# Splitting the weighted sum of a half head into two groups of six matmuls instead of three groups, in a clustered attention kernel

## The reference

```python
mask = q_assign[:, :, :, None] == k_assign[:, :, None, :]
scores = scale * np.matmul(q, k.transpose(0, 1, 3, 2))
scores = np.where(mask, scores, -1000000000.0)
scores = scores - np.max(scores, axis=-1, keepdims=True)
attn = np.exp(scores)
attn = attn / (np.sum(attn, axis=-1, keepdims=True) + 1e-09)
x = np.matmul(attn, v)          # then (token, head*dim)
h = x @ w_in;  x = (h * (1.0 / (1.0 + np.exp(-1.702 * h)))) @ w_out          # 512 -> 2048 -> 512
h = x @ w_in2; solu = h * softmax(h); out = (layernorm(solu) * g) @ w_out2   # 512 -> 1024 -> 512
```

## Time and profile before

| | |
|---|---|
| median of 3 runs | 654.56 us |
| lowest, highest | 654.29, 655.52 us |
| the profiled execution | 655.62 us, of which the span 653.8 us |
| mean granted clock of TensorE in it | 0.997 of full speed |
| busy: PE, PEld, DVE, ACT, POOL | 97%, 81%, 71%, 55%, 69% of the span |

### The profile page before, as it was taken

One profiled execution on the slowest core, in us unless ns is written; L12 is line 12 of the kernel. 1 busy time (PEld: TensorE's weight loads), 2 busy tenths in 40 slices (PEclk: granted clock), 3 DMA queues, 4 the chain that ended last, 5 costly groups with the idle time before them and its releaser, 6 DMA issues.

```text
span 653.8 us, 11249 instructions
## 1 busy us (share of the span) xinstructions
PE 632.8 (97%) x3269; PEld 531.8 (81%) x3269; DVE 465.5 (71%) x796; ACT 357.6 (55%) x712; POOL 451.1 (69%) x587
## 2 busy tenths in 40 slices
PE   7899999999999999999999999999999999999998
PEld 4488989899898988888878888788888888788876
DVE  3789999999999975646445766854556578778660
ACT  2689999999999875333334343353332154443341
POOL 3697879798798796766667777766666776857000
PEclk9989999999999999999999999999999999999999
DMA  8945454554544601233323322333330000000001
GB/s 307 288 131 140 115 146 110 144 131 107 149 118 109 227 2 65 97 97 96 96 96 96 96 90 83 94 90 93 96 96 32 1 0 18 33 18 17 33 32 49
DMA packets 26122, 62.75 MB, mean 96 GB/s; under 512 B 3697, under 2 KB 9841, under 8 KB 26097
## 3 DMA queue, kind: packets, MB, share of 16 engines
q1 hardware_dynamic: 24368, 59.30, 31.3%
q10 hardware_dynamic: 1728, 3.15, 1.3%
HBM read 46.51 MB, written 4.72 MB: 78 GB/s over the span
## 4 chain that ended last, share of the span: by engine, by line
PE 68%; ACT 11%; issue 7%; DVE 5%; POOL 4%; DMA 2%; SPq 1%; DVEq 1%; ACTq 0%; POOLq 0%
PE banks L587 7%; PE banks L602 7%; PE banks L604 7%; PE banks L603 7%; PE banks L617 7%; PE banks L619 7%; PE banks L618 6%; ACT probs L856 4%; PE banks L572 4%; ACT probs_th L867 3%; DMA pair_t<-k_t 2%; PE banks L744 2%; PE banks L742 2%; PE banks L743 2%; ACT x_sums L873 2%
## 5 line engine op out<-in xcount | busy, mean ns | idle before, releaser
L1090 DVE TENSOR_TENSOR probs_tl<-banks,probs_th 128x384 fp32r<-128x384 f32 x192 | 100.6, 547 | 10.6 <-ACT probs_th L867 7.2
L1070 DVE TENSOR_REDUCE neg_max<-banks 128x1 f32<-128x768 f32 x96 | 91.2, 950 | 6.4 <-PE banks L559 4.5
L867 ACT CAST probs_th<-banks 128x384 fp32r<-128x384 f32 x192 | 83.1, 486 | 18.8 <-PE banks L572 17.4
L1383 POOL TENSOR_TENSOR wait_scrap<-half_power 128x1 f32<-128x1 f32 x126 | 26.0, 206 | 97.3 <-PE banks L619 66.8
L856 ACT ACTIVATE probs<-banks,neg_max 128x768 f32<-128x768 f32 x96 | 88.2, 919 | 2.4 <-DVE neg_max L1070 2.3
L1459 POOL TENSOR_SCALAR probs<-probs,row_inv 128x768 f32<-128x768 f32 x96 | 87.6, 913 | 0.0
L1064 DVE TENSOR_TENSOR gl<-gate,gh 128x512 fp32r<-128x512 f32 x48 | 40.3, 840 | 63.4 <-ACT gh L841 63.4
L572 PE MATMUL banks<-ident,probs 128*128 128x128 f32 x576 | 80.0, 275 | 0.1
L587 PE MATMUL banks<-probs_th,v_parts 128*128 128x384 f32 x192 | 70.4, 366 | 9.0 <-DVE x_sums L1097 9.0
L1442 POOL TENSOR_TENSOR downl<-gelu_raw,downh 128x512 fp32r<-128x512 f32 x48 | 76.0, 1582 | 4.0
L617 PE MATMUL banks<-gh,downh 128*128 128x512 f32 x192 | 76.0, 396 | 0.4 <-POOL downl L1442 0.2
(11 more groups left out here) (166 smaller groups left out, 1431.5 us busy)
## 6 DMA issues: line engine op xcount, KB each, us to landing
gelu_raw<-w_gelu SPq DMA_DIRECT2D x48, 512.0 KB, 3.5
ln_raw<-w_ln SPq DMA_DIRECT2D x8, 512.0 KB, 4.0
pair_t<-q_t SPq DMA_DIRECT2D x4, 768.0 KB, 9.2
pair_t<-k_t SPq DMA_DIRECT2D x4, 768.0 KB, 11.6
v_raw<-v_r SPq DMA_DIRECT2D x16, 192.0 KB, 2.4
out<-gelu_raw ACTq DMA_DIRECT2D x12, 256.0 KB, 2.0
kq_raw<-k_t SPq DMA_DIRECT2D x14, 192.0 KB, 3.3
kq_raw<-q_t SPq DMA_DIRECT2D x14, 192.0 KB, 3.4
```

The lines of the kernel that those rows point to most:

```text
L867: nc.scalar.copy(probs_th[half % 2][:, c * CH:(c + 1) * CH, i * P:(i + 1) * P], pt_bank(n, c).rearrange("p (t s) -> p t s", t=CH)).then_in ...
L1070: nc.vector.tensor_reduce(out=neg_max[:, col], in_=scores[n % 2], op=ALU.max, axis=mybir.AxisListType.XY, negate=True).then_inc(max_done, 1)
L1090: nc.vector.tensor_tensor(probs_tl[half % 2][at], pt_bank(n, c).rearrange("p (t s) -> p t s", t=CH), probs_th[half % 2][at].bitcast(F32), ...
```

## The change

Two edits, both of order alone; no instruction is added or taken away.

1. The twelve matmuls come in two groups of six. The first group stands behind S_b (before: three behind S_a, five behind S_b), the second behind T_c and ahead of S_c (before: four there).
2. The first head's two transfers of cluster rows are issued ahead of the second head's two.

```diff
-            for x in range(2):
-                for j in range(2):
+            for j in range(2):
+                for x in range(2):
                     first_cluster_rows(j, x)
...
-            HEAD_SPLIT = (0, 3, 8, 12)
+            HEAD_SPLIT = (0, 6, 12)
+            HEAD_STEPS = (HEAD_LAG + AHEAD + 1, HEAD_LAG + AHEAD + 2)
+
             def head_half(it, n, c):
...
-                    for c, lag in enumerate(HEAD_LAG + AHEAD + c for c in range(3)):
-                        if c in (2,) and exists(it, n, lag, STEPS) and (n - lag) % CH == CH - 1 and not (
-                                drain and n >= lag):
-                            head_half(*lagged(it, n, lag, STEPS), c)
+                    lag = HEAD_STEPS[1]
+                    if exists(it, n, lag, STEPS) and (n - lag) % CH == CH - 1 and not (drain and n >= lag):
+                        head_half(*lagged(it, n, lag, STEPS), 1)
                     if not drain:
                         scores_of(it, n)
-                    for c, lag in enumerate(HEAD_LAG + AHEAD + c for c in range(3)):
-                        if c in (0, 1) and exists(it, n, lag, STEPS) and (n - lag) % CH == CH - 1 and not (
-                                drain and n >= lag):
-                            head_half(*lagged(it, n, lag, STEPS), c)
+                    lag = HEAD_STEPS[0]
+                    if exists(it, n, lag, STEPS) and (n - lag) % CH == CH - 1 and not (drain and n >= lag):
+                        head_half(*lagged(it, n, lag, STEPS), 0)
```

## The result

| | before | after |
|---|---|---|
| median | 654.80 us (654.29 to 655.52, 4 runs) | 659.27 us (659.09 to 659.60, 4 runs) |
| the profiled execution's span | 653.8 us | 657.0 us |
| first `x_sums` to last in the loop (28 periods) | 188.25 us | 191.38 us |
| from there to the last `x_sums` of the attention | 20.20 us | 20.67 us |

The changed kernel takes 1.0068 times as long as before (95% interval 1.0051 to 1.0085), 4.5 us more. That is slower by more than a measurement's uncertainty, and inside the range that the prediction gave to its own case (658.5 to 663 us); the 5.6 us forecast were 1.1 us too many.

A forecast was written before the change was run, and what follows sets the result against it. The prediction took a closed loop of waits in the attention, from `x_sums` to `x_sums`, as the bound. Loop 4.6 plus ends 0.4 and 0.5, with 0.05 and roundings, gave 5.6 us: 660.2 us against the median, range 656.0 to 664.0.

The forecast's parts named there:

- its own case: Whole kernel: the loop of waits lengthens and the ends add, 5.6 us slower; range 658.5 to 663 us, chance 0.70.
- The term of the loop: Attention loop: 28 periods x 0.165 us longer, 4.6 us; lower bound 3.1 us if the short offset holds in each half head.
- What bounds: Attention: one closed loop of waits from `x_sums` to the next `x_sums`, 6.70 us, sets the whole period.
- The wait that takes the place of the removed one: T_b's second group on TensorE: waits for `probs_tl` in place of `x_sums`, some 28 times, 0.5 us each.
- `x_sums` to S_b: Loop piece without the three matmuls: 1.40 to 1.51 us instead of 1.81, mean gain 0.355 us.
- S_b to S_c: Loop piece with twelve matmuls instead of nine: 3.52 us instead of 3.00, three matmuls costing 0.52 us.
- The ends: Outside the loop: first half head plus 0.4 us, last steps plus 0.52 us.
- First half head: Ahead of the loop: S_b 0.12 us earlier, three matmuls cost 0.52 us, so plus 0.4 us.
- Drain: Last attention steps: three matmuls move behind the wait that hid them, plus 0.52 us; first drained half head 0.05 us.
- Edit 2: SP's queue at the start: cost 0, the shift absorbed in a later wait; 0.57 us if that cover were gone.
- The faster case: T_b's second group finds `probs_tl` done, so the freed wait is real: 651.0 us, or 650.0 by the median; chance 0.10.
- The worse case: ScalarE's exponential holds S_b: no gain in every second half head, 665 us, or in any, 670 us; chance 0.12.

The follow-up runs named there:

- the last kernel: Kernel before, with the three matmuls put between T_b's first and second group of transposes, five behind S_b, four ahead of S_c: 648.96 us, 0.9885 of before.
- the three kernels with the changed loop: Changed kernel, 659.27 us; it with the old order of cluster rows, 659.76 us; it with old groups in first and drained half heads, 658.94 us.

## Why the prediction was right

The direction, the mechanism and the sign of each term were right, and the time is in the range. The term of the loop was half as large again as what was measured (4.6 us against 3.1), and 3.1 us is the lower bound that the prediction gave it, though not for the reason given there. Point by point:

- **What bounds.** That the loop `x_sums`, three matmuls, T_b, S_b, T_c, S_c, maximum sets the pace was read from rows that touch. `x_sums` 0.55 us or more later in it lengthened the period by 0.62 us; in the last kernel 0.30 us taken out between `x_sums` and S_b (1.51 against 1.81 in the mean) shortened it by 0.245, since 0.05 us came back between the maximum and `x_sums`.
- **The wait that takes the place of the removed one.** T_b's second group waits for `probs_tl` 28 times, 0.45 us each; forecast 28 times, 0.5. The restart price from the earlier trace rows, 0.92 us from the start of `probs_tl` to the next product, came out as 0.90 (83.35 to 84.25) and 0.92 (90.25, where the next half head's `probs_tl` starts, to 91.17).
- **`x_sums` to S_b.** Forecast 1.40 and 1.51 in turn, measured 1.36, 1.51, 1.51 and 1.36 in the four half heads of a pair; mean gain 0.376 where 0.355 was taken.
- **S_b to S_c.** Forecast 3.52, measured 3.52 in the half head shown, and 0.515 us more than before in the mean. The three matmuls cost 0.172 us each. The Trainium skill ("TensorE: Matmul & The Clock Gate", "Back-to-back issue gap") gives a stream about 131 ns for each matmul of 512 columns; the trace does not agree with it, with 0.173 us from start to start at only 384 columns.
- **The loop term was mis-sized.** Forecast 28 x 0.165 = 4.6 us, measured 191.38 - 188.25 = 3.1, that is 0.112 us a period. In the mean the pieces changed by -0.376 (`x_sums` to S_b), +0.515 (S_b to S_c), 0 (S_c to the maximum) and -0.028 us (the maximum to `x_sums`). The prediction had -0.355, +0.52, 0 and 0. The largest part of the 0.053 us is the last piece, which it took from one half head, 0.99 us, and as the same before and after. It is 0.96, 0.99, 1.05 and 0.96 us in the four half heads of a pair before, and 0.94, 0.99, 1.05 and 0.87 after. The prediction also called its 6.87 us a lower bound, since other waits can only lengthen a loop. It was none: a piece can shrink, too. In the fourth half head the maximum had just ended when `x_sums` began before, and now `x_sums` begins 0.09 us ahead of that end. ScalarE's half of the sum was done 0.42 us ahead of `x_sums` before (102.51, 102.93) and 0.68 ahead now (102.80, 103.48). Whether ScalarE had held it is open: with three between T_b's groups, `x_sums` at 94.86 starts only 0.25 us after ScalarE's half.
- **The ends.** First half head: from its S_a to its `x_sums` 6.70 us before, 7.13 after, 0.43 against 0.4 forecast. Drain: 0.47 against 0.57. 3.1 + 0.4 + 0.5 = 4.0 us. The medians differ by 4.5 (interval 3.3 to 5.6).
- **Where else it shows.** VectorE's wait for scores grew to 14.1 us; I had said 7 to 9, from a later S_c and the 2.0 us of waits for copies. VectorE is ready earlier by more than that: its last `probs_tl` ahead of the maximum ends 5.37 us after `x_sums` in the mean, before 5.58, and S_c is 0.14 us later against `x_sums`. So the gap in front of that maximum grew from 0.155 to 0.50 us. The list of waits leaves out those below 0.15 us, and half of the gaps before were shorter. The wait for copies is gone, as forecast (0.2 us, before 2.0). The MLPs kept their length: 396.2 us from the last `x_sums` to the end of the span, before and after.
- **Edit 2** cost nothing that can be measured, as forecast.
- **The rivals.** The faster case needed T_b's second group to find its `probs_tl`; it did not. The worse case, ScalarE's exponential as the gate of S_b, did not come here. With eight in the first group the exponential did hold S_b in two of the four half heads of a pair, but it cost some 0.05 us there and not the whole gain.

## What to carry to other kernels

Where several engines are each over 90% busy, look for the loop of waits whose steps touch, and price an edit by what it does to that loop; moving work out of a wait that it filled is not free even if the wait it stood behind goes with it. Check what the next instruction in the queue waits for: here it was the same engine's next result, 0.5 us behind. And if two waits of one engine follow each other, put independent work in front of each: the same three matmuls between two groups of transposes made 1.15% out of what had been a loss of 0.7%.

## What was not expected of the hardware

- VectorE's order of two operations of 0.55 us each was worth plus 3.0% in one order of TensorE and minus 0.5% in the other.
- The start scatters more than the rest of the kernel: the first scores came between 25.61 and 26.96 us over thirteen single profiles, while the period of the loop repeats within 0.01 us between the three kernels with the changed loop (6.835, 6.839, 6.841).
- A matmul of 384 columns right behind transposes took 0.25 to 0.26 us to the next start, and 0.17 us behind another one of its kind (86.65, 86.91 and 87.08 in the changed kernel).
